# Rows of the first load dealt over DRAM by their turn on the transfer engines

## What is computed

```python
kv = np.einsum('bhsd,bhse->bhde', k, v)
out = np.einsum('bhsd,bhde->bhse', q, kv)
rms = np.sqrt(np.mean(out * out, axis=-1, keepdims=True) + 1e-06)
x = (out / rms * g_norm)            # laid out as 4608 rows of 512
logits = x @ phi                    # 32 slots
d = softmax(logits, over rows);  slot_input = d.T @ x
slot_out = relu(slot_input @ w1[e]) @ w2[e]      # 8 experts, 4 slots each
result = softmax(logits, over slots) @ slot_out
```

## Time and profile before

| | us |
|---|---|
| median of 3 runs | 171.65 (171.57 to 171.8) |
| the profiled execution | 171.73 |
| its span, first to last instruction | 170.4 |
| TensorE busy in the span | 151.0 (89%) |
| ScalarE busy | 88.5 (52%) |
| VectorE busy | 86.9 (51%) |
| GpSimd busy | 59.6 (35%) |
| moved by DMA | 71.65 MB, 421 GB/s over the span |

### The profile page before, as it was taken

How to read it: one execution, slowest core, us unless ns; L and a number is a source line. 1 busy time by engine, 2 the same in 40 slices (tenths; PEclk the granted TensorE clock), 3 DMA queues, 4 the chain that set the end, 5 groups by cost and what they waited for, 6 DMA issues and landing times.

```text
span 170.4 us, 4234 instructions
## 1 busy us (share of the span) xinstructions
PE 151.0 (89%) x1834; PEld 104.0 (61%) x1834; DVE 86.9 (51%) x185; ACT 88.5 (52%) x230; POOL 59.6 (35%) x73
## 2 busy tenths in 40 slices
PE   7998998999999899999899989989999989989200
PEld 3457987979688888796696664345566533454000
DVE  1111437743677265763936798724888036319300
ACT  3015778786965887768849864202234044418300
POOL 7000247757356755366482589300000004000000
PEclk9999999999999999999999999999999999999855
DMA  5999999999999999999999999999999999999996
GB/s 193 440 435 417 478 413 409 457 430 478 419 415 439 432 441 413 419 400 460 400 458 408 448 408 423 431 458 396 431 427 431 452 435 396 427 415 439 415 447 288
DMA packets 3933, 71.65 MB, mean 421 GB/s; under 512 B 742, under 2 KB 742, under 8 KB 874
## 3 DMA queue, kind: packets, MB, share of 16 engines
q1 hardware_dynamic: 3562, 71.18, 97.8%
q0 software_dynamic: 352, 0.20, 0.4%
HBM read 61.94 MB, written 9.44 MB: 419 GB/s over the span
## 4 chain that ended last, share of the span: by engine, by line
PE 54%; DMA 16%; ACT 15%; DVE 6%; issue 1%; SPq 0%
PE psum L215 54%; DMA arena<-in_w_dram 10%; DMA arena<-in_kv_dram 6%; ACT bd L215 4%; ACT sq L215 4%; ACT xall L215 2%; DVE ms L215 2%; DVE logits L215 1%; ACT part L215 1%; ACT arena L215 1%; ACT r L215 1%; ACT d L215 1%; DVE part L215 1%; DVE acc L215 1%; DVE r L215 0%
## 5 line engine op out<-in xcount | busy, mean ns | idle before, releaser
L215 PE MATMUL psum<-bd,arena 128*128 128x192 f32 (+1 forms) x320 | 56.6, 336 | 2.4 <-ACT bd L215 1.2
L215 PEld LDWEIGHTS psum<-bd,arena 128*128 128x128 f32 (+1 forms) x320 | 45.5, 179 | 9.7 <-ACT xall L215 3.5
L215 DVE TENSOR_REDUCE ms<-sq 128x16 f32<-128x1024 f32 (+1 forms) x19 | 22.1, 1162 | 28.6 <-ACT sq L215 28.5
L215 POOL TENSOR_TENSOR part<-part,r 128x512 f32<-128x512 f32 x17 | 17.8, 1047 | 48.9 <-DVE r L215 48.9
L215 POOL TENSOR_TENSOR xall<-xall,r 128x512 f32<-128x512 f32 x34 | 34.7, 1042 | 0.0
L215 ACT ACTIVATE sq<-psum 128x512 f32<-128x512 f32 x36 | 21.5, 596 | 9.0 <-PE psum L215 8.9
L215 PEld LDWEIGHTS psum<-arena 128*64 128x64 f32 (+1 forms) x640 | 18.8, 137 | 6.6 <-issue 3.0
L215 PE MATMUL psum<-arena 128*64 128x64 f32 (+1 forms) x640 | 21.4, 226 | 0.3 <-DMA arena<-in_kv_dram 0.3
L215 ACT COPY xall<-psum 128x512 f32<-128x512 f32 x34 | 20.7, 608 | 0.0
L215 ACT COPY part<-psum 128x256 f32<-128x256 f32 (+1 forms) x38 | 13.7, 359 | 9.2 <-DVE part L215 8.0
L215 DVE TENSOR_REDUCE logits<-part 128x64 f32<-128x512 f32 (+1 forms) x18 | 17.8, 991 | 0.0
(11 more groups left out here) (80 smaller groups left out, 129.7 us busy)
## 6 DMA issues: line engine op xcount, KB each, us to landing
arena<-in_w_dram SPq DMA_DIRECT2D x4, 4096.0 KB, 23.8
arena<-in_w_dram SPq DMA_DIRECT2D x4, 2048.0 KB, 20.5
arena<-in_t_dram SPq DMA_DIRECT2D x1, 6912.0 KB, 35.6
arena<-in_w_dram SPq DMA_DIRECT2D x2, 3072.0 KB, 22.9
arena<-in_kv_dram SPq DMA_DIRECT2D x2, 2304.0 KB, 19.0
arena<-in_kv_dram SPq DMA_DIRECT2D x1, 4608.0 KB, 40.3
arena<-in_kv_dram SPq DMA_DIRECT2D x1, 3584.0 KB, 29.9
arena<-in_kv_dram SPq DMA_DIRECT2D x1, 3328.0 KB, 26.0
```

Source lines behind the costliest of these rows:

```text
L215: inst = getattr(engine, method)(*args, **kwargs)
```

## The change

The sixteen DMA engines are each taken to serve eight rows in turn. Before, the eight rows of one engine lie one behind the other in DRAM, so that the engines' first rows are 8 x 9792 = 78336 bytes apart. After, the host stores the first rows of all sixteen engines side by side, then all second rows, and so on: DRAM row 16·i + e goes to partition 8·e + i. The load's source pattern has three dimensions in place of two. Bytes, row length, destination and the number of rows stay the same.

```diff
-    nc.sync.dma_start(arena[:, : HEAD + 2304], first_in)
+    nc.sync.dma_start(arena[:, : HEAD + 2304], first_in.rearrange("(i e) n -> e i n", e=16))
...
-        "in_first_dram": first,
+        "in_first_dram": np.ascontiguousarray(first.reshape(16, 8, -1).swapaxes(0, 1)).reshape(P, -1),
```

## The result

The changed kernel takes 174.40 us (median of 6 runs, 174.2 to 174.64) against 171.73 us for the kernel before in the same job (6 runs): ratio 1.0158, 95% interval 1.0147 to 1.0169. It is slower by 2.67 us, outside the range of the prediction, on the side that had a chance of 0.15. The profiled execution took 174.64 us, with a span of 173.3 us.

The account below looks back on a forecast made before the run. The prediction took the never-idle DMA engines, the latest one setting the end, as the bound; +0.12 (issue) - 0.10 (first rows) + 0.03 (later rounds) = +0.05 us on the median of 171.65 gave 171.70 us, range 171.15 to 172.1.

Parts of the forecast that it names:

- What bounds the kernel: Whole kernel: the sixteen DMA engines never run out of work from 2.55 to 160 us; the latest engine sets the end.
- Time lost or won on the first load is not absorbed anywhere later: From first load to end: what the latest engine is late by at 5.7 us it is late by at 170 us.
- TensorE's restart on kv0: Sign at 11.21 us, plus or minus 0.3: if it moves and the end doesn't, the forecast is wrong.
- The landing is covered for 0.6 us: First load's landing: TensorE is in fillers until 6.78 us, so some 0.6 us of later landing cost nothing.
- Issue: SP's issue of the first load: longer for the added source dimension, +0.12 us, bounds -0.04 and +0.58 us.
- rival B: First entry of SP's queue: issue becomes the bound, up to +0.58 us, 172.26 us; chance 0.15 with any other such loss.
- First rows: First row of each engine in the first load: excess time could go, at most -0.71 us; taken as -0.10 us.
- Later rounds: First load's rows after the first: neighbouring rows read at once could lose 0.06 us; half taken, +0.03 us.
- bytes, rows and destination are unchanged: First load's transfers: 128 rows, eight to an engine, at 0.37 us in the steady rounds; effect nothing.
- Rival C: First load: engines' rows aren't side by side in time, so only the longer issue is paid; 171.77 us, chance 0.12.
- The rule on split descriptors: First load's rows: descriptors starting off a 256-byte boundary fetch unused bytes; some 0.03 us on four engines over the load.

Follow-up runs that it names:

- the run with fillers: The changed kernel with two more wide filler matmuls on TensorE ahead of the first product: 174.32 us, ratio 1.0145 to the kernel before.
- the load of two pieces: The kernel before with each first-load row as two 4896-byte pieces in DRAM, a third dimension, partitions still outermost: 172.36 us, ratio 1.0044.

## Why the prediction was wrong

*What bounds the kernel* was right, and the experiments rest on it: 1.27 us of arithmetic won moved the end by nothing that can be measured, and 2.9 us lost on the first load's and kv0's rows are 2.9 us of span.

*But not every difference counts.* "Time lost or won on the first load is not absorbed anywhere later" holds for the loss. The 0.33 us by which the plain load with near rows was read earlier was absorbed, by 149 us. That is a sign that the prediction had named for itself: TensorE's restart on kv0 moved and the end did not, "for then the queue does run dry somewhere". The stretch from 140 to 150 us is where the lead goes.

*The landing is covered for 0.6 us*: right, and too little for a load that came 3.18 us later. TensorE went idle, which the prediction had not allowed for; by the run with fillers it cost nothing that can be measured at the end.

*Issue*: the term was taken as +0.12 us between -0.04 and +0.58 us. It measured 0.72 - 0.38 = +0.34 us, inside the bounds, at the very point from which rival B was to decide. Alone, in the load of two pieces, the third dimension cost 0.70 us of time (ratio 1.0024 to 1.0063).

*First rows*: taken as -0.10 us. In the changed kernel they take 0.70 us each, for a mean of 0.83 us before, and what that won is lost in the rounds behind them. That rows near each other in DRAM shorten the start is not shown: 0.33 us in one execution of the plain pattern is less than the 0.40 us by which one and the same load was read apart in two kernels.

*Later rounds* is the step that failed. It read: "if every row came to cost what the dearest of these rounds shows, 0.378 for 0.369 us, seven rows would add 0.06 us. I take half, +0.03 us." Measured: 0.72 us a row from the third round on, some six times 0.35 = 2.1 us, and 1.08 for 0.65 us on the first rows of kv0 behind them. The bound was taken from rows that all belong to loads of one shape. It looked only at where the rows come from, DRAM, and held "bytes, rows and destination are unchanged" for an answer on where they go. The destination as a whole is unchanged; which of its partitions are written at the same moment is not.

*Why the rate is halved.* A load of partitions 0 to 63 runs at 0.77 us a row, two loads of 0 to 31 and of 96 to 127 at 0.67 us, one of 32 to 95 at 0.37 us, the plain one of all 128 at 0.37 us. So the rate goes by which partitions a load writes: those on one side of 64 alone are slow, and 64 that lie half below and half above are not. The Trainium skill, page "SBUF — State Buffer", section "Door 1: The DMA port swizzle", has a rule that gives this: a port is chosen by bits 2 to 4 and bit 6 of the partition number, so 0 to 63, like 0 to 31, reach eight of sixteen ports. The trace agrees, with 0.77 against 0.37 us. By this rule 32 to 95 reach all sixteen, which the run of 0.37 us bears out.

For the changed load the rule gives the following. If the pattern is split over sixteen engines by its slowest dimension, engine e serves partitions 8e to 8e + 7 in turn. At each moment the sixteen engines then write partitions 8e + i, which by the rule lie on eight ports, two engines to each; twice 0.37 is 0.74 us, and 0.72 us was seen. No row of a trace names the engine of a row, so this sharing-out is inferred from the rates. The pattern with seven partitions to an engine fits it: by the same count at least twelve of the sixteen engines are alone on a port at any moment, and its rows took 0.54 us, between 0.37 and 0.72 us.

*Rival C* had named the point, but not its price. It cites the page "DMA: Bandwidth & Descriptors" of the Trainium skill, section "The descriptor swizzle", by which an engine of a plain load of 128 rows serves two groups of four partitions. That puts each engine on a port of its own, and full rate is what the plain load shows. The prediction took from it only that the first rows would not be side by side, and priced it at the issue alone. Read together with the port rule it says the opposite of harmless: a pattern that makes the hardware share the rows out in another way gives up one port to one engine. The rule on split descriptors that the prediction weighed from the Trainium skill, at an estimate of 0.03 us there, has no effect that can be measured beside the loss.

## What to carry to other kernels

A load's pattern decides not only what is read but which partitions the sixteen engines write at one moment. Keep the 128 partitions as the slowest dimension on both sides: with another dimension outermost the same 128 rows of 9792 bytes went at 224 instead of 423 GB/s, and the same happens to plain loads of partitions 0 to 63. Of the cuts tried here only the part with partitions 32 to 95 kept the full rate (0.37 us a row); the rest of that load, 0 to 31 and 96 to 127, did not, so no cut by partitions is shown that keeps it for a whole load. A cut along the rows keeps all 128 partitions in each part, as this kernel's own loads of batch 0 do: 423 GB/s in the first and 431 in the second. And before pricing a changed pattern ask of its destination, too, what each engine does at the same moment.

## What was not expected of the hardware

A third dimension in a load's pattern raises SP's issue from 0.38 to 0.70 to 0.72 us, in every kernel that had one for all 128 rows. Reading near rows of DRAM from all engines at once costs nothing (0.376 us a row at 10 KB apart). In that kernel the rows also overlap, so that fewer different bytes are read; rows that lie near and don't overlap were tried in the dealt patterns alone, where they ran at 0.37 us on partitions 32 to 95. Padding the changed kernel's rows to a 256-byte boundary changed nothing that can be measured (ratio 1.0154 against 1.0158).
